# A fused attention and two-mixer kernel: first batch reordered, four loops unrolled, preparation for the third stage moved

## What is computed

```python
kv = einsum('bhsd,bhse->bhde', k, v); out = einsum('bhsd,bhde->bhse', q, kv)
x = out / sqrt(mean(out*out, -1) + 1e-6) * g_norm        # then (B, S=576, 512)
theta = x @ w_theta                                      # 512 x 512
y = w_tok_r @ (x*cos(theta)) + w_tok_i @ (x*sin(theta))  # over the 576 tokens
u = x + y;  x2 = u + maximum(u @ w_ch, 0)                # 512 x 512
h = maximum(x2^T @ w_tok1, 0) @ w_tok2                   # 576 -> 256 -> 576
u2 = x2 + h^T;  result = u2 + maximum(u2 @ w_ch1, 0) @ w_ch2   # 512 -> 1536 -> 512
```

## Time and profile before

| | |
|---|---|
| median of 3 runs | 1187.77 us (1186.92 to 1188.11) |
| the profiled execution | 1189.02 us, of which the span of its records is 1187.2 us |
| PE busy, of the span | 1160.4 us (98%) |
| PE's weight loads | 1120.1 us (94%) |
| DVE, ACT, POOL busy | 850.6, 480.4, 330.0 us |
| chain that ended last | PE 65%, issue 15%, POOL 9%, DVE 6%, DMA 3%, ACT 2% |

### The profile page before, as it was taken

How to read it: one execution, slowest core, us unless ns; L and a number is a source line. 1 busy time by engine, 2 the same in 40 slices (tenths; PEclk the granted TensorE clock), 3 DMA queues, 4 the chain that set the end, 5 groups by cost and what they waited for, 6 DMA issues and landing times.

```text
span 1187.2 us, 20987 instructions
## 1 busy us (share of the span) xinstructions
PE 1160.4 (98%) x7790; PEld 1120.1 (94%) x7790; DVE 850.6 (72%) x1243; ACT 480.4 (40%) x758; POOL 330.0 (28%) x210
## 2 busy tenths in 40 slices
PE   6999999999999999999998999999999999999998
PEld 5899999999899999899997999999999999999998
DVE  3977879797978878677564676666666786666664
ACT  3623324151424233234442455555556543333331
POOL 4462525444452524231551222223200000000000
PEclk9999999999999999999999999999999999999999
DMA  9614525151625230319996787766858999999983
GB/s 287 189 26 102 120 72 127 48 130 21 159 40 155 44 80 0 83 41 310 355 314 210 242 308 277 268 231 252 292 227 313 389 312 299 251 256 311 291 201 54
DMA packets 327245, 228.14 MB, mean 192 GB/s; under 512 B 231312, under 2 KB 295184, under 8 KB 326160
## 3 DMA queue, kind: packets, MB, share of 16 engines
q1 hardware_dynamic: 324784, 227.03, 62.6%
q10 hardware_dynamic: 2400, 0.30, 0.2%
HBM read 136.84 MB, written 92.80 MB: 193 GB/s over the span
## 4 chain that ended last, share of the span: by engine, by line
PE 65%; issue 15%; POOL 9%; DVE 6%; DMA 3%; ACT 2%; SPq 0%; POOLq 0%; DVEq 0%; ACTq 0%
PE bank L1368 9%; PE bank L1370 9%; PE bank L1369 9%; PE bank L43 7%; PE bank L45 7%; PE bank L44 7%; PE bank L371 4%; PE bank L365 4%; PE bank L366 4%; POOL z_z L956 3%; PE bank L310 2%; POOL z_z L958 2%; DMA z_g<-g_scratch 1%; POOL tokens_x_token_major L949 1%; POOL weights_rms_inverse L941 1%
## 5 line engine op out<-in xcount | busy, mean ns | idle before, releaser
L365 PE MATMUL bank<-weights_tok,z_z 128*128 128x288 f32 x576 | 165.0, 301 | 1.0 <-ACT z_z L591 1.0
L366 PE MATMUL bank<-weights_tok,z_z 128*128 128x288 f32 x576 | 161.3, 294 | 0.0
L371 PE MATMUL bank<-weights_tok,z_z 128*128 128x288 f32 x576 | 125.7, 296 | 1.1 <-POOL z_z L958 0.6
L365 PEld LDWEIGHTS bank<-weights_tok,z_z 128*128 128x128 f32 x576 | 108.1, 188 | 3.2 <-ACT z_z L591 2.4
L366 PEld LDWEIGHTS bank<-weights_tok,z_z 128*128 128x128 f32 x576 | 108.2, 188 | 0.0
L371 PEld LDWEIGHTS bank<-weights_tok,z_z 128*128 128x128 f32 x576 | 92.5, 187 | 3.0 <-POOL z_z L961 2.1
L941 POOL TENSOR_TENSOR weights_rms_inverse<-weights_mean_squares,weights_minus_half 128x8 f32<-128x8 f32 x40 | 65.5, 1639 | 95.2 <-DVE weights_mean_squares L724 95.1
L956 POOL TENSOR_TENSOR z_z<-tokens_cos,z_z 128x512 fp32r<-128x512 f32 x24 | 32.0, 1331 | 184.2 <-ACT z_z L589 184.2
L596 ACT ACTIVATE weights_x_channel_major<-attention_u 128x288 fp32r<-128x288 f32 x64 | 28.5, 445 | 126.0 <-DVE attention_u L791 126.0
L43 PE MATMUL bank<-weights_x_channel_major,weights_ch 128*128 128x288 f32 x256 | 77.3, 302 | 0.0
L45 PE MATMUL bank<-weights_x_channel_major,weights_ch 128*128 128x288 f32 x256 | 75.4, 294 | 0.0
(11 more groups left out here) (297 smaller groups left out, 3639.2 us busy)
## 6 DMA issues: line engine op xcount, KB each, us to landing
g_scratch<-attention_staged SPq DMA_DIRECT2D x36, 960.0 KB, 4.3
weights_g<-g_scratch SPq DMA_DIRECT2D x24, 1152.0 KB, 10.3
g_scratch<-attention_staged SPq DMA_DIRECT2D x36, 384.0 KB, 4.8
x_scratch<-attention_u SPq DMA_DIRECT2D x8, 1152.0 KB, 4.5
u_scratch<-attention_u SPq DMA_DIRECT2D x8, 1152.0 KB, 7.5
weights_raw_u<-u_scratch SPq DMA_DIRECT2D x6, 1536.0 KB, 7.6
qkv_u_left<-u_scratch SPq DMA_DIRECT2D x12, 768.0 KB, 9.5
x_tokens_scratch<-z_x_turned SPq DMA_DIRECT2D x112, 72.0 KB, 2.0
```

Of the source, the lines that this page charges most:

```text
L365: pe.matmul(out, x, wtok[0][:, zt, hs], start=(i == 0), stop=False)
L366: pe.matmul(out, x, wtok[1][:, zt, hs], start=False, stop=False)
L371: mm = pe.matmul(tok_bank(b, g)[:, 0:HALF], z[1][:, zt, c * P:(c + 1) * P], wtok[0][:, zt, half * HALF:(half + 1) * HALF], start=False, st ...
```

## The change

The first batch of phase A gets a new order on all engines. PE runs 24 identity transposes before its first product. K and V of six heads are loaded first, then their left rows, the first query tile, and K and V of the last two heads; the other query tiles come ahead of the theta weights, the token weights behind them. `norm` writes straight into `x_token_major`; the norm weight is applied as a per-row factor (`gain_col`) in `x_hi` and `x_lo`, and in place by POOL (`gain_in_place`) for `rotate`. Token weights use four banks, and all of them are transposed behind the first theta tiles. Attend and squares use more banks.

In later batches `attend(b+1, 0)` moves ahead of the last pair, two of four `turn_q` move into the batch before, and `norm` stands ahead of `residual`. ACT's and DVE's loop of phase A and PE's and DVE's loop of phase B are written out. The load of `raw_u` moves from turn 4 to turn 5 of SP, behind the store of batch 5; `prep_hi(FIRST)` moves from batch 5 to 6, and SHARED to 7. In phase D `seed_e(0, 1)` moves ahead of `c22(0, 0)` and `split`.

```diff
@@ sync, phase A
-        for part in range(2):
-            heads = slice(part * HP, (part + 1) * HP)
-            load_heads(kin, k, 0, heads, s_kv0[part])
-            load_heads(vin, v, 0, heads, s_kv0[part])
-        load_left(kin, k, 0, s_kv0[2])
-        load_left(vin, v, 0, s_kv0[2])
+        early, late = slice(0, 2 * (HP - 1)), slice(2 * (HP - 1), H)
+        load_heads(kin, k, 0, early, s_kv0[0])
+        load_heads(vin, v, 0, early, s_kv0[0])
+        load_left(kin, k, 0, s_kv0[1])
+        load_left(vin, v, 0, s_kv0[1])
+        load_query_tile(0, 0, s_q0[0])
+        load_heads(kin, k, 0, late, s_kv0[2])
+        load_heads(vin, v, 0, late, s_kv0[2])
+        load_query_tile(0, 1, s_q0[1])
@@ tensor, phase A
+        pe.wait_ge(s_ident, 2)
+        for _ in range(WARM_UP):
+            pe.transpose(ps_acc[0][:, 0:P], ident[:, :], ident[:, :])
         pe.wait_ge(s_zero, 2)
+        kv_part(0, 0)
+        kv_part(0, 1)
         q_transpose(0, 0)
+        kv_part(0, 2)
         attend(0, 0)
+        for j in range(1, NT - 1):
             q_transpose(0, j)
+            attend(0, j)
         x_transpose(0, 0)
+        q_transpose(0, NJ)
+        attend(0, NJ)
+        x_transpose(0, 1)
+        theta_part(0, 0, 0)
+        theta_part(0, 0, 1)
+        x_transpose(0, 2)
+        theta_part(1, 0, 0)
+        theta_part(0, 1, 0)
+        theta_part(1, 0, 1)
+        theta_part(1, 1, 0)
+        tok_weight(0)
+        tok_weight(1)
+        x_transpose(0, 3)
+        x_transpose(0, 4)
+        theta(0, 2)
+        tok_weight(2)
+        tok_weight(3)
+        theta(0, 3)
+        tok_weight(4)
+        tok_weight(5)
+        theta(0, 4)
+        for i in range(NT + 1, 2 * NT + 2):
+            tok_weight(i)
...
-                if first and pair == 1:
+                if pair == (1 if first else NJ - 1):
                     attend(b + 1, 0)
@@ scalar, phase A (after q_copy(0, 3), squares(0, 2))
+        q_copy(0, 4)
         x_hi(0, 0)
+        squares(0, 3)
+        theta_weight_hi(0)
+        x_hi(0, 1)
         theta_weight_hi(1)
+        squares(0, 4)
+        x_hi(0, 2)
+        tok_weight_hi(0)
+        tok_weight_hi(1)
+        x_hi(0, 3)
+        x_hi(0, 4)
+        sines(0, 0)
...
+        tok_weight_hi(6)
+        tok_weight_hi(7)
+        sines(0, 2)
+        for i in range(8, 2 * NT + 2):
+            tok_weight_hi(i)
@@ vector, phase A
+        norm(0, 4)
+        x_lo(0, 3)
+        fraction(0, 0)
+        magnitude(0, 0)
+        x_lo(0, 4)
         tok_weight_lo(0)
         tok_weight_lo(1)
+        fraction(0, 1)
...
+        tok_weight_lo(10)
+        tok_weight_lo(11)
+        rotate(0, 2)
...
                 if more:
-                    turn_q(b + 1, 0)
-                    turn_q(b + 1, 1)
+                    for hp in range(0 if b == 1 else EARLY_TURNS, HP):
+                        turn_q(b + 1, hp)
                 rotate(b, NJ)
...
+                if more and g > NC:
+                    norm(b + 1, g - NC)
                 residual(b, g)
...
-        loop(dve, body, 1, B - 1)
+        for b in range(1, B - 1):
+            body(b)
@@ phase B
+            if n == B - 3:
+                sp.wait_ge(g_w, len(UP_ORDER))
+                sp.wait_ge(s_st, (B - 4) * DMA)
+                nxt["load"](sp, 0)
...
-    PREP_HI = {B - 3: [FIRST], B - 2: [SHARED], B - 1: [MIDDLE, SECOND]}
-    PREP_LO = {(B - 3, 4): FIRST, (B - 2, 4): SHARED, (B - 1, 2): MIDDLE, (B - 1, 4): SECOND}
+    PREP_HI = {B - 2: [FIRST], B - 1: [SHARED, MIDDLE, SECOND]}
+    PREP_LO = {(B - 2, 5): FIRST, (B - 1, 2): MIDDLE, (B - 1, 4): SECOND}
@@ vector, phase D
+            if g == 0:
+                seed_e(g, 1)
+            else:
                 seed_e(g, 0)
             c22(g, 0)
             split(M + 7)
-            seed_e(g, 1)
+            if g > 0:
+                seed_e(g, 1)
```

More of the change, by code:

```diff
@@ L266, in tensor, with kv_part @@
     def tensor(pe, nxt):
+        KV_PARTS = [(range(HP - 1), range(NJ)), (range(HP), [NJ]), ([HP - 1], range(NJ))]
+        def kv_part(n, part):
+            first = isinstance(n, int) and n == 0
+            if first:
+                pe.wait_ge(s_kv0[part], 2 * DMA)
+            pairs, js = KV_PARTS[part]
+            for j, hp, side in itertools.product(js, pairs, range(2)):
+                h, apart = 2 * hp + side, first and hp == HP - 1
+                bank = ps_kv_late if apart else ps_kv
+                if apart:
+                    start, stop = part == 1, part == 2 and j == NJ - 1
+                else:
+                    start = part == 0 and j == 0 and hp == 0
+                    stop = part == 1 and hp == HP - 2 if first else part == 2 and j == NJ - 1
+                mm = pe.matmul(bank[side * D:(side + 1) * D, hp * D:(hp + 1) * D], kin[:, h, j, :],
+                               vin[:, h, j, :], start=start, stop=stop)
+            if part == 1 and first:
+                mm.then_inc(p_kv_early, 1)
+            if part == 2:
+                mm.then_inc(p_kv, 1)
         def kv(n):
             wait(pe, s_kv, KV_LOADS * DMA * n)
-            wait(pe, kv_placed, 4 * n)
+            wait(pe, kv_placed, 4 * n + 2 if not isinstance(n, int) or n > 0 else 0)
             wait(pe, a_xhi, NT * n)
             wait(pe, d_xlo, NT * n)
[L273 to L283, removed]
+            for part in range(len(KV_PARTS)):
+                kv_part(n, part)
         def q_transpose(n, j):
@@ L904, in body @@
                     mean_square(b + 1, g - 3)
-                if more and g >= 4:
-                    norm(b + 1, g - 4)
+                if more and g == NC:
+                    norm(b + 1, 0)
             u_lo(b, NG - 1)
@@ L913, in body @@
                     norm(b + 1, NT - 1)
+                if 1 <= g <= EARLY_TURNS and 1 <= b < B - 2:
+                    turn_q(b + 2, g - 1)
                 if more and g == 5:
@@ L973, in gpsimd @@
         gp.wait_ge(s_ident, 4)
-        gp.wait_ge(s_raw[1], DMA)
         def attention(n):
@@ L981, in attention @@
                     gain(n, j - 1)
-        attention(0)
+        for j in range(NT):
+            inverse_rms(0, j)
+        gp.wait_ge(s_raw[1], 3 * DMA)
+        for j in range(NT):
+            gain_in_place(j)
         def body(b, more=True):
@@ L1173, in tensor @@
         hidden(0)
-        def body(n):
+        for n in range(B - 1):
             mix(n)
             hidden(n + 1)
-        body(0)
-        loop(pe, body, 1, B - 1)
         mix(B - 1)
@@ L1266, in batch @@
                 x_lo(dve, n + 1, 0)
+            else:
+                nxt["prep_lo"](dve, 0, SHARED)
             for g in range(NG):
@@ L1277, in body @@
             batch(2 * pair + 1, 1, pair)
-        body(0)
-        loop(dve, body, 1, PAIRS - 2)
-        body(PAIRS - 2)
+        for pair in range(PAIRS - 1):
+            body(pair)
         batch(B - 2, 0, PAIRS - 1)
```

260 lines of the change are left out of this document (147 added, 113 removed).

## The result

The changed kernel takes 1190.5 us (median of 15 runs, 1187.9 to 1193.7) against 1187.6 us before (15 runs, 1185.7 to 1189.4): ratio 1.0026, 95% interval 1.0018 to 1.0035. It is slower; 1178.3 was forecast, and 1190.5 lies outside the range of 1172 to 1185. Stages are compared between these two traces.

What follows compares the result with a forecast made beforehand. PE was taken to bound the kernel, busy 1160.4 of 1187.2 us. Seam 6.9, VectorE's loop 1.0, phase D 1.3, batches 3.2, less the opening's 2.9, made 9.5: 1187.77 to 1178.3 us, range 1172 to 1185.

Steps and rivals of the forecast that it cites:

- step 1 of the opening: Opening loads: K, V, left rows and first query tile there at 11.6 us, attend(0, 0) at 12.8.
- Steps 2 to 5: Opening from attend(0, 0) at 12.8: theta at 25.8, fraction(0, 0) at 34.8, VectorE's last weight part at 54.4 us.
- step 5: Opening, fraction(0, 0) to last weight part: VectorE takes 17.8 us plus 1.8 of waits, ending 54.4 against 51.55, 2.9 later.
- the opening pays: Rival: the theta lead of 4.8 us reaches the token mix, 17.2 us won in all, 1170.6; chance 0.17.
- step 2: Opening's query tiles: a chain of 2.3 us each, first products at full clock, x_transpose(0, 0) at 20.7 us.
- the clock falls again: Rival: PE drops to half clock in the opening between kv products and first attends, costing 2.8 us, 1181.1; chance 0.14.
- The seam: Before phase C: moving the FIRST split and writing out PE's loop removes stall, slow clock and loop gap; worth 6.9 us.
- PE's loop exit: Seam term at batch 7: PE's 1.44 us wait on leaving its loop, 1.6 with overlap, goes when written out.
- Batches: Batches 1 to 6: attend moved ahead of the last token-mix pair and norm ahead of residual fill bubbles; worth 3.2 us.
- VectorE's loop exit: Start of batch 7: VectorE's 2.73 us wait behind its loop goes when written out; worth 1.0 us of PE.
- phase D: seed_e(0, 1) ahead of a split of 2.54 us removes PE's wait; worth 1.3 us.
- The slower side: Rival: written-out batches stall instruction fetch at each new stretch of code, 12 us in six batches, 1190.3; chance 0.05.

Runs made afterwards that it cites:

- e3: Changed kernel with the three norm-weight loads on ACT's queue held back until the first K and V have landed; 1186.4 us, ratio 0.9992.
- e10: Changed kernel with only the two norm-weight column loads held back until K and V landed, broadcast row still first on ACT's queue; 1191.0 us, ratio 1.0034.
- e12: Kernel of e10 with the norm-weight broadcast row issued first on SyncE's queue ahead of K; 1189.3 us, ratio 1.0012.
- e13: Changed kernel whose first load on ACT's queue reads 128 different rows of q, real norm-weight loads after K and V; 1188.3 us, ratio 1.0006.
- e14: Kernel before, its only edit the norm-weight broadcast row issued first on ACT's queue; 1191.5 us, ratio 1.0028.
- e4: Changed kernel with the last two heads of K and V loaded ahead of left rows and first query tile; 1190.0 us, ratio 1.0023.
- e11: Kernel of e3 with x_transpose(0, 3) and x_hi(0, 3) ahead of two token-weight parts on PE and ACT; 1185.6 us, ratio 0.9986.
- e5: Kernel of e3 with VectorE's fraction(0, 0) and magnitude(0, 0) ahead of x_lo(0, 3); 1185.6 us, ratio 0.9983.
- e6: Kernel of e3 with 1 warm-up identity transpose in place of 24; 1186.8 us, ratio 0.9993.
- e1: Kernel before with every part of the change but the new first batch; 1181.0 us, ratio 0.9945.
- e2: Kernel of e1 with batches 1 to 6 in their old order; 1183.2 us, ratio 0.9963.
- e7: Kernel of e1 with norm(b+1, 0) ahead of mean_square(b+1, 1) in VectorE's order; 1180.1 us, ratio 0.9937.
- e8: Kernel before with only the moved load and splits of raw_u, every loop kept; 1182.7 us, ratio 0.9962.
- e9: Kernel of e7 with batch 1 in its old order and phase B's loops kept; 1178.0 us, ratio 0.9931.

## Why the prediction was wrong

**The step that failed is step 1 of the opening.** It read "at the 251 GB/s of the first 20 us that is 2.1 us: 11.6 ... attend(0, 0) at 12.8" and put the load of the norm-weight row at nothing, though the change moves it from behind K and V to the very start. By bytes it is nothing: 32 KB of 2.6 MB. But A0 came at 18.00, 5.2 us late, and 4.25 of these go when the three norm-weight loads wait for K and V (e3: 13.75). The row alone makes 3.95 of them (e10: 17.70); e12, e13 and e14 show the same row at work on the other queue, other rows doing no harm in its place, and the kernel before losing 3.7 us at the token mix by it. The other 1.0 us is mostly the last piece of V, which step 1 had landed at 11.6; its products start at 12.40 in e3, after a wait of 0.36 for that load.

**Steps 2 to 5 were right**, as distances: the token mix stands 41.8 us behind A0 in the forecast (54.6 - 12.8), after the change, and in e4, e10, e11 and e12. In e3, e5, e6 and e13, where the clock fell on the way, it stands 43.1 to 45.4 behind. (The terms of step 5 as printed add up to 18.0, not 17.8.) So the opening would cost 2.9 us with A0 at 12.8, and costs 3.9 with the norm-weight loads out of the way in e11 (55.65 against 51.76). The rival "the opening pays" is dead: in no variant of the new opening did the token mix come before 55.6. With the opening's whole miss of 5.2 us taken off, the change would still stand near 1185.3; the second term that failed is that of the batches, below.

**"The warm-up products end before K and V arrive and cost nothing; what they buy is in step 2"**: true as far as it goes. With K and V 5.7 us later the clock fell again before the kv products; with K and V soon behind it, the warm-up is worth about 1 us (e6).

**The rival "the clock falls again"** happened, at places that changed from run to run: 10 to 16 us and 62 to 64 after the change (the granted clock is 0.50 in both), 38 to 42 in e3, 14 to 28 in e5. I gave it 0.14. It is no exception: the mean granted clock is 0.993 to 0.996 in all 15 executions of the changed kernel, and 0.999 or 1.000 in all 32 of e1, e2, e7, e8 and e9, which keep the old opening. Its price was forecast as 2.8 us; e5's trace took 18.25 us from the first attend to the first theta product in place of 12.9, so 5.3 were lost there. In the changed kernel's own trace neither fall cost much: behind the first PE still had to wait 0.17 us for the last piece of V at 16.64, and with the second in it batch 0 takes 67.16 us, against 67.18 in e3, which has no fall there.

**The seam was right in total (e8: 6.4, e9: 6.9; forecast 6.9), but one of its terms had a wrong cause.** The 1.6 us of PE's loop exit went with the moved load and did not need the written-out loop: e8 keeps the loop and has no gap; e14, the kernel before, keeps loop and stall (3.3 us) and has it (1.3). Whether the gap would come with the stall and no loop, no run shows. That the term came true is luck: the change did both. By the Trainium skill (Runtime: NRT & Kernel Launch, Instruction fetch mechanics) I had put both exits down to a branch whose target must be fetched. VectorE's 2.73 and 2.61 us with the loop, and none without, agree; PE's exit in e8, with the loop and without a gap, does not. In the changed kernel itself 5.7 of 6.9 arrived; of the other 1.2, 0.8 are the wait for VectorE's residuals at `mix(5)`, 1.18 us where before it was 0.38, and the rest has no single row. These waits for residuals are not steady: the nine traces with this seam and the new opening have 1.0 to 3.0 us of them, and the stage takes 145.4 to 148.0 us (e5, e3). `raw_u` landed with 2.5 us of ACT's time to spare (2.6 forecast).

**Batches: 3.2 us forecast, next to nothing arrived** (+0.26 over batches 1 to 5; in batch 6 the new order gave 0.55, 62.36 us in e2 against 61.81 in e1). The mechanism was right: the old bubbles went. The size was wrong: 0.7 a batch was forecast, and batches 2 to 5 went from 64.69 to 64.51. Three things were not seen. `attend(b+1, 2)` moved up into the shadow of `norm(b+1, 0)`; I wrote that norm goes ahead of residual, but not that tile 0's norm still stood behind tile 1's mean squares (e7 removes the wait and wins 0.15). Batch 1 costs 0.98, not 0.4 (e9 takes it back). And written-out loops cost 0.3 a batch in the old order (e2 against e8). In e2 another of VectorE's 0.46 us subtractions than before meets POOL's product and takes 1.59; that this is the reason is argued, not shown.

**VectorE's loop exit** gave 0.8 of the 1.35 us of batch 6 (63.17 before, 62.36 in e2; 1.0 forecast), **phase D** 0.8 (1.3).

The slower side was given 0.06. Its mechanism there, stalls of written-out code, did not happen: PE and VectorE have no wait without a releaser left. I had no rival in which a small load that is moved to the front of a queue holds up the large ones.

## What to carry to other kernels

When a transfer is moved, price it by what runs beside it in its new place, and not by its bytes: a one-row broadcast of 32 KB belongs behind the loads that the first product waits for. Write a serial opening as distances from the first attend; they held to 0.1 us wherever the clock held, while its start was off by 5. And before a wait without a releaser is blamed on a loop, look whether a stall stands in front of it: take the stall away first and see what stays.

## What the runs showed of the hardware

- A load that reads one 256-byte row of DRAM 128 times, issued first of all, kept the transfers of the core at 48 and 66 GB/s between 2 and 4 us in the new opening (e10, e12), where 229 and 236 is the rate without it (e13, e3), and at 102 in place of 223 in the old one (e14). K and V of 1.5 MB then let the first products start at 11.16 (SyncE's queue) or 11.83 (ACT's) in place of 8.70 and 8.26, 2.5 to 3.6 us later. What it blocks is open, and so is what it costs behind K and V, where no run takes it away.
- The same gap of PE can cost its clock or not: 2.64 us idle for `fraction(0, 0)` brought the granted clock to 0.51 in e3, and left it at 1.00 in the changed kernel; 2.38 us ahead of the token mix did the opposite in these two.
- A window can read 1.00 while PE runs at half pace: in the kernel before, half an attend took 1.06 us until 17 us, with 1.00 in every window. e8 has the same code there, took 0.61, and had its token mix at 50.47 in place of 51.76. So an opening is compared by the duration of its products, and 51.76 itself moves by over 1 us between executions.
- A wait without a releaser can be the echo of a stall: PE's gap of 1.44 us at `mix(7)` stood 18 us behind the stall, came with it in e14, and went with it in e8.
